# In the loop of routed loads, the request for the second matrix moves ahead of the request for the first

## What is computed

```python
# 1. a recurrent attention over B=4, H=8, S=768, D=40 -> x (3072 x 320)
# 2. dense layer
h = x @ w_in                       # 320 x 2048
g = np.where(h >= 1, h, np.where(h <= -1, 0.0, (h + 1) ** 2 / 4))
x = g @ w_out                      # 2048 x 320
# 3. routed layer, E = 8 experts, each token goes to one
expert_idx = np.argmax(x @ w_gate, axis=1)
for e in range(E):
    h = np.maximum(x[mask_e] @ w1[e], 0.0)     # 320 x 1024
    out[mask_e] = gate_w[mask_e, None] * (h @ w2[e])   # 1024 x 320
```

## Time and profile before

| | before |
|---|---|
| median of 3 runs | 823.09 us (822.97 to 824.31) |
| profiled execution, its own time | 822.7 us |
| its span, first to last instruction | 820.8 us |
| PE busy | 764.8 us (93%) |
| DVE busy | 593.6 us (72%) |
| ACT busy | 423.7 us (52%) |
| POOL busy | 322.6 us (39%) |
| DMA queue of SP | 87.46 MB, 34.1% of 16 engines |

### The profile page before, as it was taken

One profiled execution on the slowest core, in us unless ns is written; L12 is line 12 of the kernel. 1 busy time (PEld: TensorE's weight loads), 2 busy tenths in 40 slices (PEclk: granted clock), 3 DMA queues, 4 the chain that ended last, 5 costly groups with the idle time before them and its releaser, 6 DMA issues. The chain is left out here.

```text
span 820.8 us, 17200 instructions
## 1 busy us (share of the span) xinstructions
PE 764.8 (93%) x5765; PEld 743.4 (91%) x5765; DVE 593.6 (72%) x1006; ACT 423.7 (52%) x649; POOL 322.6 (39%) x297
## 2 busy tenths in 40 slices
PE   2788999999999999999999999999849999999994
PEld 1788999999999999999999999989849999999994
DVE  4653868787878787887878888668647676867850
ACT  3023445454545454545455455646645676757751
POOL 3352543534343545444454534550723323232111
PEclk9999999999999999999999999999988999999998
DMA  7962232222222322232233200544887535545300
GB/s 213 301 166 75 77 91 76 91 75 91 74 91 77 95 83 94 88 95 83 92 92 96 78 16 1 183 117 97 264 308 238 184 109 192 164 151 169 116 20 5
DMA packets 41458, 97.05 MB, mean 118 GB/s; under 512 B 6936, under 2 KB 24482, under 8 KB 39755
## 3 DMA queue, kind: packets, MB, share of 16 engines
q1 hardware_dynamic: 37498, 87.46, 34.1%
q0 software_dynamic: 3920, 9.08, 3.9%
HBM read 105.63 MB, written 9.33 MB: 140 GB/s over the span
## 5 line engine op out<-in xcount | busy, mean ns | idle before, releaser
L545 POOL TENSOR_TENSOR g_t<-u_t,r_t 128x512 f32<-128x512 f32 x96 | 135.9, 1416 | 254.6 <-ACT u_t L695 254.5
L690 ACT ACTIVATE r_t<-bank,neg 128x512 f32<-128x512 f32 x96 | 66.0, 688 | 186.6 <-PE bank L1388 186.6
L1400 PE MATMUL bank<-wo_h,g_h 128*128 128x328 f32 x384 | 127.2, 331 | 0.0
L1002 DVE TENSOR_SCALAR u_t<-bank 128x512 f32<-128x512 f32 x96 | 66.1, 689 | 75.3 <-ACT r_t L690 47.5
L1400 PE MATMUL bank<-wo_h,g_l 128*128 128x328 f32 x384 | 120.1, 313 | 0.0
L1400 PE MATMUL bank<-wo_l,g_h 128*128 128x328 f32 x384 | 120.1, 313 | 0.0
L627 POOL DMA_INDIRECT out_x<-ob,idx_tok x31 | 39.2, 1264 | 157.6 <-ACT ob L765 153.3
L695 ACT ACTIVATE u_t<-u_t,half 128x512 f32<-128x512 f32 x96 | 69.4, 723 | 40.6 <-DVE u_t L1002 38.7
L938 DVE TENSOR_TENSOR_SCAN W<-W,cst 128x512 f32<-128x512 f32 x48 | 83.2, 1737 | 4.4 <-DMA W<-decays 4.4
L1521 PE MATMUL bank<-w_h,h_h 128*128 128x320 f32 x248 | 79.1, 319 | 3.7 <-DVE w_l L1063 2.6
L1388 PE MATMUL bank<-xT_h,wi_h 128*128 (+1 forms) x384 | 78.8, 287 | 1.6 <-issue 1.6
(11 more groups left out here) (231 smaller groups left out, 1947.1 us busy)
## 6 DMA issues: line engine op xcount, KB each, us to landing
raw<-in_w SPq DMA_DIRECT2D x12, 1280.0 KB
W<-decays SPq DMA_DIRECT2D x24, 512.0 KB, 5.3
raw<-in_w SPq DMA_DIRECT2D x12, 1024.0 KB
raw2n<-in_w SPq DMA_DIRECT2D x7, 1280.0 KB
raw1n<-in_w SPq DMA_DIRECT2D x7, 1024.0 KB
raw<-in_w SPq DMA_DIRECT2D x24, 256.0 KB
qG<-in_q SPq DMA_DIRECT2D x24, 180.0 KB
qT<-in_qt SPq DMA_DIRECT2D x48, 80.0 KB
```

What stands on the lines that cost most here:

```text
L545: pool.tensor_tensor(g_t[p % 2][:, :], u_t[p % 2][:, :], r_t[p % 2][:, :], ALU.add).then_inc(sm["g_done"], 1)
L690: act.activation(r_t[p % 2][:, :], bank_h[p % 2][:, :], ACT.Relu, bias=neg1[:, 0:1]).then_inc(sm["r_done"], 1)
L1002: dve.tensor_scalar(u_t[p % 2][:, :], bank_h[p % 2][:, :], 1.0, -1.0, ALU.min, ALU.max).then_inc(sm["u_done"], 1)
L1400: mm = pe.matmul(bank_acc[tt][:, 0:DL], l[p % 4][:, c], r[:, f, :], start=f == 0 and a == 0, stop=f == NT1 - 1 and a == 2)
```

## The change

Two lines of the SP program change places. Within each pass of the loop the call for the second matrix of slot s - 1 comes first and the call for the first matrix of slot s second. Both calls keep their own waits, their register loads and their DMAs. Nothing else in the program differs.

```diff
             refill2(2)
             refill2(3)
             for s in range(5, NS):
+                refill2(s - 1)
                 refill(s)
-                refill2(s - 1)
             for s in (NS - 2, NS - 1):
```

## The result

| | before | after |
|---|---|---|
| median | 823.03 us (4 runs, 822.71 to 824.31) | 834.0 us (4 runs, 833.92 to 834.29) |
| ratio, 95% interval | | 1.0119, 1.0103 to 1.0135 |
| profiled execution, its span | 822.7, 820.8 us | 834.29, 832.4 us |
| PE busy | 764.8 us | 767.8 us |

What follows compares the result with a forecast made beforehand. PE was taken as the bound, busy 182.68 of 184.00 us in the loop's rounds. Terms 9.5 + 2.1 + 0.1 = 11.7 us on 822.7 gave 834.4, plus 0.4 for the median: 834.8 us, range 831.5 to 839.0.

Steps and rivals of the forecast that it cites:

- The second matrix's request gains nothing at issue: SP in every pass: it already waited for the second matrix's buffer, so that request leaves when it left before.
- Slot 11: Pass s = 10: its first matrix lands at 700.4 us, so PE stalls 9.5 us, between 8.1 and 11.9.
- The transfer model: Slots 11 and 12: transfer starts 1.6 us after the request at 688.6; both matrices take 10.2 us at full use.
- The clock: After slot 11's stall PE runs at the lower clock for a while, costing 2.1 us, between 1.2 and 3.1.
- the half of the Trainium skill: Rule for the slow clock: the penalty is half the slow stretch's duration; the sum would be 0.3 us higher.
- Slot 8: Pass s = 7: its skipped request goes later, conversion begins at 651.0 us; PE loses 0.1 us, between 0 and 0.6.
- Rival (b): Slot 8: a false-condition DMA's flag rises only behind the transfer ahead; 5.2 us more, 839.9 us, chance 0.12.
- Slot 16: Pass s = 14: its first matrix lands at 752.6 us against conversion at 751.31, costing PE 0.
- (a): Slot 11: the stall comes but the clock stays up; 9.6 us lost, 832.7 us, chance 0.10.
- (c): Slot 11: its matrix lands by 690.9 us, so PE would not wait at all; 823.1 us, chance 0.05.
- (d): The loop: second matrices land earlier and PE's short waits go, at most 1.3 us; 821.8 us, chance 0.03.

Runs made afterwards that it cites:

- experiments 3 and 4: New order, but in pass 10 first matrix requested before second, after waiting for second's buffer: 830.49 us; 4 also waits until first landed before requesting second: 830.91 us.
- experiment 2: The two calls change places in every pass except s = 10, against the kernel before: 822.39 us, ratio 0.9992.
- experiment 6: New order with slot 8's first matrix, normally skipped, always loaded: 845.33 us, ratio 1.027 to the kernel before.
- experiment 1: The two calls change places in pass s = 10 alone, against the kernel before: 833.68 us, ratio 1.0134.
- experiments 8 and 9: Kernel before with calls ahead of loop reordered, slot 4's second matrix first; 8 also has new order in pass 5: 820.87 us (repeat 822.39); 9 not: 822.68 us.

## Why the prediction was right

*The second matrix's request gains nothing at issue.* Right: 648.14 and 688.02 for 648.39 and 688.58. The lead of 0.3 and 0.6 us is mostly the whole program's, which ran 0.3 us ahead there. The count of waits behind it, 12 of 12, was misread: the loop makes 13 such calls, and one did not wait, that of pass 15 (issued at 753.20 us in the kernel before, one set of register loads behind the first matrix). After the change all 13 waited. The sum does not depend on it.

*Slot 11.* First matrix asked for about 690.4 (689.85), in use at 700.4 (700.78), PE back at 707.3 (707.66), stall 9.5 us (10.01). The transfer model, both matrices together 10.2 us at full use, gave the time to half a microsecond, but partly by luck. All but two packets of slot 11 had landed at 698.66, and the last two, which ended at 700.33, came behind an instruction packet that the model doesn't have; without it the conversion would have begun at about 699.1 and the stall been 8.3 us (an estimate: 1.7 less), near the lower bound of 8.1. The model was also simpler than the truth: experiments 3 and 4 gave 9.5 and 8.4 us for a first matrix with nothing ahead of it, where I counted 7.4. For the forecast that did not matter, as slot 11's was the last of the two to be asked for, and only the pair's total counted. The Trainium skill, "DMA: Bandwidth & Descriptors", section "Queues, rings and completion order", has the descriptors of one ring consumed in order. The trace agrees: in the kernel after, the first packet of slot 11's matrix started at 692.91, when the last ones of slot 12's second matrix were starting (693.35). That what is behind doesn't count fits experiments 3 and 4, one profile each.

*The clock.* Forecast 2.1 us. The parts p = 2 and p = 3 took 6.41 us where full speed takes about 4.1, so 2.3, and the windows give 2.0. PE worked at 0.50 from 707.66 to 713, for 5.3 us; the clock had fallen while PE stood (0.50 already from 703 to 704). At full speed the matmuls of line 1468 start 0.12 us apart (698.12 and 698.24 before), at the lower clock 0.21 (709.94 and 710.15 after), so each slow microsecond costs 0.44, and 5.3 of them 2.3. By the half of the Trainium skill ("TensorE: Matmul & The Clock Gate", section "HAM oscillation — how this bites in real kernels") this would be 2.7; the measured 2.3 stands. Against the kernel before at the same place it is less. There the two parts held a wait of 0.34 us that the slower PE no longer has. From the start of p = 2 to the first instruction behind p = 3 it took 4.5 us before (697.82 to 702.31) and 6.25 after (707.66 to 713.91), so 1.8:

```profile
702.31 0.27 PE L1436 MATMUL bank<-cst,xg 128*128 128x128 f32 x1
```
```profile
713.91 0.28 PE L1436 MATMUL bank<-cst,xg 128*128 128x128 f32 x1
```

*Slot 8.* Conversion forecast for 651.0, seen at 650.69, no stall (0.1 forecast). Rival (b), that skipped requests queue, is refuted by the trace: the third was issued at 650.56 and ACT began at 650.69, while the second matrix of slot 9 was on its way (its packets ran from 648.98 to 654.40). The window of those 0.7 us has a DMA share of 0.93:

```profile
650.00:650.70 0.70, 0.70 (x7) 0.70 (x7) 0.00 (x0) 0.01 (x1) 0.00 (x0) 1.00 0.93 395
```

*Slot 16.* A wait of 0.60 us on ACT, hidden, where I had 1.3.

*Rivals.* (a) fell, since the clock did drop. (c) and (d) would have needed slot 11's matrix by 690.9; it came 9.9 us after. (d)'s possible gain was tested by experiment 2, where eleven passes in the new order brought 0.9992 with the interval over 1.

The sum of the terms, 11.7, compares with 11.6 between the spans and 11.0 between the medians. The 11.6 are complete at the first instruction behind the two parts (713.91 against 702.31): p = 2 of slot 10 came 9.8 us later (707.66 against 697.82), and the two parts took 1.8 longer. The stall of PE reads 10.0 and not 9.8 because PE had run 0.2 to 0.3 us ahead until then (part p = 0 of slot 10 at 693.59 against 693.91). So the wait was forecast some 0.3 to 0.5 us too small and the clock 0.3 too large, and the two errors cancel.

## What to carry to other kernels

In a queue that waits in program order, the place of a request is set by two times: when its buffer falls free and when its data is first used. Putting a request with much slack ahead of one with none costs its wait, its issue and its bytes. Here 6.3 us were the wait. Issue and bytes had part in the other 5.1, but how large a part is not shown. Look for the pair with no slot between them, since only those passes decide, and compute the stall from a place in the same trace where the load already came late. And a gain at one load can come back as a wait at the next one behind it: read the waits of both matrices after each move.

## What the runs showed of the hardware

A DMA issued with a false condition raised its flag within about 0.1 us of its issue (650.56 to 650.69), past 1280 KB under way on the same queue. Two register loads from SBUF and their bookkeeping on SP cost 1.5 us before a DMA, after the change too (648.35 to 649.91, 688.26 to 689.85); with one register load it was 0.85 us (650.30 to 651.15, experiment 6).

A packet that loads instructions (16 KB, 1.2 us) was under way when the end of slot 11's load came in, in each of the three kernels with this stall of about 10 us. In the kernel after and in experiment 1 the last two packets ended 1.7 us behind all the others (700.33 against 698.66, 701.20 against 699.53); in experiment 6 the last part of the flag came 0.9 us behind the last packet (710.64 against 709.71).

The load of slot 5 took from 7.5 to 12.2 us from request to use under the same calls (experiments 8 and 9), and from 10.0 to 13.6 in the eight kernels, the one before among them, that have the old calls ahead of the loop. So a single profile of a stretch in which loads, gathers and scatters meet tells little, whereas slot 11's stall came out as 10.01, 10.03 and 9.60 us in three kernels.
